# Attention, gated product and mixture of experts: nine branch bodies in the place of three for the second part of the experts' first product

## What is computed

```python
def _moe2_ref(x, w_gate, w_noise, noise, w1, w2):
    # x (2304, 512), w1 (8, 512, 1024), w2 (8, 1024, 512)
    noisy_logits = x @ w_gate + np.log1p(np.exp(x @ w_noise)) * noise
    top2 = np.argpartition(-noisy_logits, 2, axis=1)[:, :2]
    top2_w = softmax of the two logits
    for e in range(E):
        for k in range(2):
            mask = top2[:, k] == e
            h = np.maximum(x[mask] @ w1[e], 0.0)
            out[mask] += top2_w[mask, k, None] * (h @ w2[e])
```

## Time and profile before

| what | value |
|---|---|
| median of 3 runs | 1040.43 us (1039.68 to 1040.98) |
| the profiled execution's own time | 1039.33 us |
| its span, first to last instruction | 1037.5 us |
| mean granted clock of TensorE | 0.994 |

### The profile page before, as it was taken

How to read it: one execution, slowest core, us unless ns; L and a number is a source line. 1 busy time by engine, 2 the same in 40 slices (tenths; PEclk the granted TensorE clock), 3 DMA queues, 4 the chain that set the end, 5 groups by cost and what they waited for, 6 DMA issues and landing times.

```text
span 1037.5 us, 16723 instructions
## 1 busy us (share of the span) xinstructions
PE 1014.1 (98%) x5934; PEld 932.5 (90%) x5935; DVE 444.2 (43%) x935; ACT 369.6 (36%) x683; POOL 529.5 (51%) x416
## 2 busy tenths in 40 slices
PE   7899999999999999999999999999999999999996
PEld 6899999878989898989898999889898989898985
DVE  6788888773214232433335753222222323222221
ACT  6999988852213131322223413112120212121110
POOL 8689999520000202020202227968788887877742
PEclk8999999999999999999999999999999999999998
DMA  8688886383960101010402175362627162634303
GB/s 174 158 199 204 202 207 170 96 278 102 370 255 1 61 0 61 0 61 0 143 1 93 41 250 138 120 145 88 165 59 197 18 206 58 192 71 142 41 9 43
DMA packets 73986, 124.97 MB, mean 120 GB/s; under 512 B 13377, under 2 KB 30913, under 8 KB 73938
## 3 DMA queue, kind: packets, MB, share of 16 engines
q1 hardware_dynamic: 65218, 104.05, 33.9%
q0 software_dynamic: 8640, 20.00, 9.5%
q10 hardware_dynamic: 80, 0.29, 0.1%
HBM read 78.73 MB, written 36.67 MB: 111 GB/s over the span
## 4 chain that ended last, share of the span: by engine, by line
PE 74%; DVE 1%; issue 0%; POOLq 0%; ACT 0%; DVEq 0%
PE ps_turn L1711 13%; PE ps_x L1687 10%; PE ps_b L1687 10%; PE ps_x L1776 10%; PE ps_a L1758 9%; PE ps_b L1758 9%; PE ps_small L1711 8%; PE ps_a L1667 2%; PE ps_small L1659 1%; PE ps_turn L1649 1%; PE ps_small L1641 0%; POOLq L966 0%; PE ps_turn L1799 0%; PE ps_small L1642 0%; DVE y_tile L1452 0%
## 5 line engine op out<-in xcount | busy, mean ns | idle before, releaser
L1214 POOL DMA_INDIRECT expert_rows<-x_rows,slot_idx x36 | 41.7, 1158 | 306.1 <-DVE slot_idx L1587 296.9
L1271 POOL DMA_INDIRECT out<-y_tile,out_rows x40 | 63.2, 1579 | 76.6 <-DVE y_tile L1452 72.2
L1314 ACT CAST xT_high<-ps_a 128x512 fp32r<-128x512 f32 x40 | 23.3, 587 | 190.1 <-PE ps_a L1667 190.1
L1389 ACT COPY prod<-ps_a 128x384 f32<-128x384 f32 x48 | 23.0, 480 | 162.1 <-PE ps_b L1758 162.1
L1594 DVE TENSOR_TENSOR prod<-ps_b,prod 128x384 f32<-128x384 f32 x48 | 26.8, 557 | 123.9 <-ACT prod L1389 123.9
L1687 PE MATMUL ps_b<-xT_high,w_high 128*128 128x256 f32 (+3 forms) x256 | 77.5, 303 | 0.0
L1711 PE MATMUL ps_turn<-wo_high,hT_high 128*128 128x512 f32 x192 | 76.2, 397 | 1.1 <-issue 1.1
L1687 PE MATMUL ps_x<-xT_high,w_high 128*128 128x256 f32 (+3 forms) x256 | 77.0, 301 | 0.0
L1687 PE MATMUL ps_x<-xT_high,w_low 128*128 128x256 f32 (+3 forms) x256 | 76.9, 300 | 0.0
L1687 PE MATMUL ps_x<-xT_low,w_high 128*128 128x256 f32 (+3 forms) x256 | 76.9, 300 | 0.0
L1687 PE MATMUL ps_b<-xT_low,w_high 128*128 128x256 f32 (+3 forms) x256 | 76.8, 300 | 0.0
(11 more groups left out here) (272 smaller groups left out, 3009.9 us busy)
## 6 DMA issues: line engine op xcount, KB each, us to landing
spare<-e_w SPq DMA_DIRECT2D x16, 1024.0 KB, 5.2
w_raw<-e_w SPq DMA_DIRECT2D x16, 1024.0 KB, 8.6
expert_rows<-zeros SPq DMA_DIRECT2D x8, 1290.0 KB, 15.8
ex_rows<-expert_rows SPq DMA_DIRECT2D x40, 258.0 KB, 4.0
k_raw<-kT SPq DMA_DIRECT2D x31, 288.0 KB, 4.8
out<-zeros SPq DMA_DIRECT2D x11, 512.0 KB, 10.5
q_raw<-qT SPq DMA_DIRECT2D x16, 288.0 KB, 4.8
q_mix<-q_top SPq DMA_DIRECT2D x16, 288.0 KB, 3.7
```

What stands on the lines that cost most here:

```text
L1214: nc.gpsimd.indirect_dma_start(out=rows_dram, out_offset=bass.IndirectOffsetOnAxis(ap=slot_idx[:, k, t:t + 1], axis=0), in_=x_rows[:, t, : ...
L1271: nc.gpsimd.indirect_dma_start(out=out, out_offset=bass.IndirectOffsetOnAxis(ap=out_rows[:, j:j + 1], axis=0), in_=y_tile[j][:], in_offset ...
L1314: nc.scalar.copy(xT_high[:, :, j * P:(j + 1) * P], ps_xT[j % XS][:].rearrange("p (c t) -> p c t", t=P)).then_inc(xhigh, 1)
L1389: nc.scalar.copy(prod[f % 2][:], ps_a[f % 2][:, 0:G]).then_inc(a_copied, 1)
```

## The change

The list of widths becomes 512 to 640 in steps of 16, so that there are nine branch bodies where three were, in the loop and in the last stretch. The index of the width is found by comparing the rows left with all eight narrower widths and adding up, in two operations over 16 x 8 elements and a copy; these now stand behind the step that raises `planned`, and raise a semaphore of their own, `widths_known`, on which TensorE waits ahead of the load of the index.

```diff
--- before.py
+++ after.py
@@ -11,7 +11,7 @@
 ACT = mybir.ActivationFunctionType
 AX = mybir.AxisListType
 STRETCH = 640
-WIDTHS = (576, 608, 640)
+WIDTHS = (512, 528, 544, 560, 576, 592, 608, 624, 640)
 META = 4
 SUMS = 9
 KEPT_AT, KEPT = 86016, 12288
@@ -1000,7 +1000,7 @@
         slot_idx = sb("slot_idx", [P, 2, TT], mybir.dt.int32)
         G1 = plan[1].shape[1]
         plan_room = {k: sb(f"plan_{k}", [P, n]) for k, n in
-                     (("each", E * max(G1, E + 1, REGION // STRETCH)), ("of_stretch", G1), ("first_row", G1), ("expert_of", G1),
+                     (("each", max(E * max(G1, E + 1, REGION // STRETCH), G1 * (len(WIDTHS) - 1))), ("of_stretch", G1), ("first_row", G1), ("expert_of", G1),
                       ("held", E), ("bounds", E + 1), ("stretches", E), ("unused", E), ("added", E))}
 
         const_loaded = sem("const_loaded")
@@ -1079,6 +1079,7 @@
         rows_read = sem("rows_read")
         rows_known = sem("rows_known")
         planned = sem("planned")
+        widths_known = sem("widths_known")
         block = ctx.enter_context(nc.Block())
 
         srcs = [(w1, MC, ew1_high, ew1_low), (w2, FC, ew2_high, ew2_low)]
@@ -1475,7 +1476,7 @@
                 second_low_part(3)
                 low_h(0, 6, PARTS_FIRST)
                 low_h(0, 7, PARTS_FIRST)
-                plan_experts(nc, dve, plan_step, planned, counts, consts, C, REGION, plan, plan_room)
+                plan_experts(nc, dve, plan_step, planned, widths_known, counts, consts, C, REGION, plan, plan_room)
                 for j in range(AHEAD, TILES):
                     low_x(0, j)
                 for j in range(AHEAD - 1):
@@ -1730,6 +1731,7 @@
                     return first_stretch()
                 pe.wait_ge(weights_cut, 2 * CUTS * before + CUTS)
                 first_product(g, before, 0)
+                pe.wait_ge(widths_known, 1)
                 step = pe.value_load(widths_i[0:1, bass.ds(g, 1)], min_val=0, max_val=len(WIDTHS) - 1)
                 for k, width in enumerate(WIDTHS):
                     with pe.If(step == k):
@@ -1839,7 +1841,7 @@
     return add_up, each, across, along
 
 
-def plan_experts(nc, dve, step, planned, counts, consts, C, REGION, plan, room):
+def plan_experts(nc, dve, step, planned, widths_known, counts, consts, C, REGION, plan, room):
 
 
 
@@ -1851,6 +1853,8 @@
     number = consts[:, C["stretch"]:C["stretch"] + G]
     starts = consts[:, C["start"]:C["start"] + E]
     limits = consts[:, C["limit"]:C["limit"] + K]
+    W = len(WIDTHS) - 1
+    narrower = consts[:, C["width"]:C["width"] + W]
     ones = consts[:, C["ones"]:C["ones"] + E - 1]
     earlier = consts[:, C["earlier"]:C["earlier"] + (E + 1) * E].rearrange("p (a b) -> p a b", b=E)
     of_stretch, first_row, expert_of, held, bounds, stretches, unused, added = (
@@ -1878,12 +1882,11 @@
     add_up(number, bounds[:, 1:E], added[:, 0:E - 1], ALU.is_ge, of_stretch)
     link(nc.vector.tensor_scalar(of_stretch, of_stretch, counts[:, 0:1], None, ALU.add))
     link(nc.vector.tensor_tensor(rows_left[:], of_stretch, first_row, ALU.subtract))
-    link(nc.vector.tensor_scalar(of_stretch, rows_left[:], float(WIDTHS[1]), None, ALU.is_gt))
-    link(nc.vector.scalar_tensor_tensor(out=of_stretch, in0=rows_left[:], scalar=float(WIDTHS[0]), in1=of_stretch, op0=ALU.is_gt, op1=ALU.add))
-    link(nc.vector.tensor_copy(widths_i[:], of_stretch))
-
     link(nc.vector.scalar_tensor_tensor(out=first_row, in0=number, scalar=bounds[:, E:E + 1], in1=first_row, op0=ALU.is_lt, op1=ALU.mult))
     nc.vector.tensor_copy(first_rows_i[:], first_row).then_inc(planned, 1)
+    link(nc.vector.tensor_tensor(each(G, W), along(rows_left[:], W), across(narrower, G), ALU.is_gt))
+    link(nc.vector.tensor_reduce(of_stretch, each(G, W), AX.X, ALU.add))
+    nc.vector.tensor_copy(widths_i[:], of_stretch).then_inc(widths_known, 1)
 
 
 def bass_attention_moe(nc, qT, kT, v, w1, w2, w3T, w_out, w_gate_noise, noise, e_w1, e_w2, const_in, rows_q, rows_k, C, out):
@@ -1981,7 +1984,7 @@
     limits = [*range(0, N, STRETCH)]
     tiles = STRETCH // P
     widths = (("ident", P), ("before", P), ("ones", P), ("expert", E), ("start", E), ("stretch", max_stretches + 1), ("zero", 1),
-              ("limit", len(limits)), ("token", N // P), ("place", tiles), ("nowhere", tiles), ("earlier", (E + 1) * E))
+              ("limit", len(limits)), ("width", len(WIDTHS) - 1), ("token", N // P), ("place", tiles), ("nowhere", tiles), ("earlier", (E + 1) * E))
     C, at = {}, 0
     for name, width in widths:
         C[name] = at
@@ -1994,6 +1997,7 @@
     const[:, C["start"]:C["start"] + E] = np.arange(E) * region
     const[:, C["stretch"]:C["stretch"] + max_stretches + 1] = np.arange(max_stretches + 1)
     const[:, C["limit"]:C["limit"] + len(limits)] = limits
+    const[:, C["width"]:C["width"] + len(WIDTHS) - 1] = WIDTHS[:-1]
     const[:, C["token"]:C["token"] + N // P] = np.arange(N).reshape(N // P, P).T
     const[:, C["place"]:C["place"] + tiles] = np.arange(STRETCH).reshape(tiles, P).T
     const[:, C["nowhere"]:C["nowhere"] + tiles] = N + np.arange(STRETCH).reshape(tiles, P).T
```

## The result

The changed kernel takes 1157.09 us (median of 6 runs, 1155.59 to 1162.25) against 1040.06 us: ratio 1.113, 95% interval 1.1115 to 1.1146. It is 117 us slower. The forecast was 1063 us with a range to 1154, so the sign was right, and the size and the range were missed. The rival that the loop is fetched anew in each pass had 1155 us.

The account below looks back on a forecast made before the run. TensorE, busy 98% of the span, was taken to bound the kernel. Columns -3.84, code-fetch stalls +21.5 and clock +5 sum to +22.7 us, from the 1040.4 median to 1063 us; range 1050 to 1154, the forecast's own 1052 to 1075.

Parts of the forecast that it names:

- The rival that the loop is fetched anew in each pass: TensorE's loop code doesn't stay held, so jumps in passes 2 to 6 wait as in pass 1: 1155 us, chance 0.33.
- Passes 2 to 6: Loop passes after the first: all ten code blocks taken to stay held, so nothing added to the time.
- Pass 1: First loop pass: code-fetch stalls at both ends of the branch, 6.2 us ahead of the body and 6.2 behind.
- Last stretch: Written-out stretch after the loop: code-fetch stalls of 1.1 us ahead of its body and 9.5 us behind.
- the rival's walk: Block-by-block count of fetch waits in passes 2 to 6 if nothing stays held, with jumps back: 77 us.
- The fetch time of 4.2 us: Time taken for one dependent fetch of a TensorE code block, of which queued instructions cover some 3.1 us.
- The columns: Second part's matmuls: 96 rows less of width in all, 0.64 us per 16, so 3.84 us removed.
- The plan: Three operations leave the road to `planned`, about 0.6 us sooner; gains nothing, and the new wait costs nothing.
- The other end: Rival that fetches don't string: stalls stay at 1.1 and 0.5 us, total 1036.6 us; chance 0.06.
- The clock: Granted clock falling behind three long TensorE stalls: 1.7 us each, 5 us; the fetched-anew rival adds some 15 us.
- The jumps: Rule weighed: about 108 ns per compare-and-branch, nine come to 1 us a stretch, hidden by the queue; kernel 3.84 us sooner.
- The range: 1050 to 1154 us: the forecast's case and about three quarters of the fetched-anew rival's.

Follow-up runs that it names:

- six bodies: Widths 544, 560, 576, 592, 608, 640 in place of the changed kernel's nine, in loop and last stretch: 1110.79 us, ratio 1.0676.
- five bodies: Widths 544, 560, 592, 608, 640 in place of the changed kernel's nine, in loop and last stretch: 1044.99 us, ratio 1.0049.
- the nine walked in threes: The changed kernel's nine bodies with compares in two levels, so groups of three are jumped over as a whole: 1116.91 us, ratio 1.0749.
- the old widths: The changed kernel with nine bodies at widths 576, 608 and seven times 640, so six bodies never run: 1194.66 us in a single run.

## Why the prediction was wrong in size

**The step that failed** is "Passes 2 to 6": "If all stay held, as those of before do, nothing is added: the value taken, since these rows are the nearest." Ten blocks don't stay; each pass fetched 10 or 11. The rows were the nearest but lay on the other side of a limit: they showed five blocks and the one asked for ahead held, and the loop was to lie on ten. The rule of the Trainium skill, "Advanced Engine Details and Errata", section ISA Cache (128 KB on TensorE, lines of 16 KB, that is eight), was named in the rival and given 0.33; the runs with five and six bodies agree with it to the block, and with it the rival should have been the forecast. The same section also says "Only 2 cache lines!"; for TensorE the runs contradict that, since a loop on five blocks and one on seven (five bodies) ran passes 2 to 6 without a packet.

**Step by step**, idle us between matmuls, predicted and measured. Pass 1: 6.2 and 6.27 ahead of the body, 6.2 and 7.81 behind it. Last stretch: 1.1 and 2.21, 9.5 and 8.18. Passes 2 to 6, as the rival's walk had them with 1.1 for the jump back: 14.8 and 16.6; 16.3 and 11.8; 16.8 and 13.9; 12.6 and 14.0; 16.8 and 14.1. The sum of all seven is 100.3 against 94.9. That the rival's 1155 us come within 2 us of 1157 is in part luck: its idle time is 5.4 us too long and its clock term, 20 us, 7.9 too small. The fetch time of 4.2 us was somewhat long for a string of fetches: in 646.8 to 656.3 of the changed kernel q8 brings

```profile
q8 instruction: 4, 0.07, 2.5%
```

four packets, which begin 3.1 us apart.

**The columns** fell by 96, stretch by stretch as worked out, 3.84 us. **The plan** costs nothing (1.0002). **The other end**, that the fetches don't wait for one another, is refuted by the stalls of pass 1. **The clock**: 5 us in the forecast, 20 in the rival; 27.9 measured. Most of the gap is that the forecast had three stalls to charge for; the middle of 1.7 us a stall was too little besides. Counted from stretch 1's first matmul, and with idle time and columns taken off, the clock cost 27.6 us with 12 stalls of over 2 us in the changed kernel, 22.2 with 10 with six bodies, 21.8 with 10 for the nine walked in threes, and 16.8 with 7 for the old widths: 2.2 to 2.4 us a stall, whether the stalls had 5 us in the mean or 20. Over the stretches the granted clock was 0.88 to 0.93 where it had been 1.00; the last stretch's chain shows 7.97 and then 5.44 us for the same 24 matmuls, the former in part at 1.2 GHz and the latter at 2.4, and those just behind a stall are the slow ones.

**The jumps** themselves: the rule weighed there (a compare-and-branch of about 108 ns, the Trainium skill, "Advanced Engine Details and Errata", Control Flow Timing) isn't contradicted, since with five bodies passes 2 to 6 have no idle time at all with up to five compares each (TensorE is busy for all 280 us from 694 to 974); it just isn't what a jump costs when its target has to be fetched.

**The range** ended at 1154 and missed 1157 by little; it cut off a part of the rival's own band (1120 to 1160), which held a third of the chance.

Left open: whether the block given up is the one fetched or the one entered longest ago (both give the same packets here), and the waits longer than the walk's in three kernels (54 us against 38, 58 against 40 to 55, 140 against 110 to 120), though it had the packets of every kernel right. A computed jump to the body, with a hint ahead of it or without, was written but has no measurement, and a body short enough to loop over the eight blocks of features was not tried.

## What to carry to other kernels

Count the instructions of a loop's pass, branch bodies that aren't taken included, and lay them on the blocks in which code is fetched, before working out what a branch saves: here 1,531 instructions stayed held and 1,734 cost 66 us more. Count blocks, with the one asked for ahead, and not bytes. A chain of `If` bodies is walked block by block even where nothing in it runs, and a body written out in code that runs once pays too; so place few widths well rather than many, and group the tests so that whole groups are jumped over. Where the nearest rows lie below the size that the change makes, they are no evidence that the same holds above it.

## What the runs showed of the hardware that I had not expected

The step from held to not held is sharp: 33 packets with five bodies, 79 with six, 94 with nine. One body of 202 instructions over the limit makes the whole loop be fetched in every pass, not the part that doesn't fit: the 45 packets beyond the 34 that a single walk through the program would bring are nine in each of passes 2 to 6, its eight blocks and the one asked for ahead. The half clock was paid by the stall, 2.2 to 2.4 us each, not by the stall's length. And the same 94 packets cost 95 us of idle time or 140, by where in the chain the body taken stands.
